# The head of a three-stage kernel: gate weights as 128x32 tiles, loads in another order, four banks, and the softmax split among other work

## The reference, cut to what matters

```python
# 1: pooled attention over q, k, v: (8, 8, 576, 64), k and v averaged over 8 neighbouring rows
scores = scale * q @ k_p.T;  attn = softmax(scores);  x = attn @ v_p      # x as (4608, 512)
# 2: gated product with w1, w2 (512 x 1024), w3 (1024 x 1024), w_out (1024 x 512)
a = x @ w1;  b = x @ w2
x = (a * b @ w3) @ w_out
# 3: routed experts: 8 experts, w1 (512 x 1024), w2 (1024 x 512) each
logits = x @ w_gate + modality_bias[modality_id]                          # w_gate (512 x 8)
e_idx = argmax(logits);  gate_w = the softmax's largest value
out[mask e] = gate_w * (relu(x[mask e] @ w1[e]) @ w2[e])
```

## Time and profile before

| | us |
|---|---|
| median of 3 runs | 1252.79 (1251.92 to 1253.19) |
| the profiled execution's own time | 1254.1 |
| its span, first to last instruction | 1252.3 |
| first matmul of the head | 7.24 |
| first product with w1, end of the head | 98.86 |
| PE busy | 1213.1 (97% of the span) |
| DVE, ACT, POOL busy | 549.8, 284.3, 207.5 |

### The profile page before, as it was taken

How to read it: one execution, slowest core, us unless ns; L and a number is a source line. 1 busy time by engine, 2 the same in 40 slices (tenths; PEclk the granted TensorE clock), 3 DMA queues, 4 the chain that set the end, 5 groups by cost and what they waited for, 6 DMA issues and landing times.

```text
span 1252.3 us, 26312 instructions
## 1 busy us (share of the span) xinstructions
PE 1213.1 (97%) x10372; PEld 1158.8 (93%) x10373; DVE 549.8 (44%) x1299; ACT 284.3 (23%) x647; POOL 207.5 (17%) x242
## 2 busy tenths in 40 slices
PE   7899999999999999999999999999999999999996
PEld 6789989999999999999999999989989989999995
DVE  2774655636546546557455143542222234222221
ACT  2432222312222312222222123311211122111110
POOL 1333012102210111121020000022112112112121
PEclk9989999999999999999999999999999999999998
DMA  5752103213223023022030004025111111111111
GB/s 206 267 174 83 71 36 92 81 44 82 85 67 119 27 83 108 19 86 95 27 100 1 36 1 168 27 68 185 51 42 52 40 34 52 34 42 59 34 51 34
DMA packets 41812, 92.75 MB, mean 74 GB/s; under 512 B 9587, under 2 KB 16755, under 8 KB 40692
## 3 DMA queue, kind: packets, MB, share of 16 engines
q1 hardware_dynamic: 32868, 66.68, 16.1%
q0 software_dynamic: 6400, 20.50, 5.1%
q10 hardware_dynamic: 2448, 4.21, 1.1%
HBM read 70.88 MB, written 21.01 MB: 73 GB/s over the span
## 4 chain that ended last, share of the span: by engine, by line
PE 93%; DVE 3%; DMA 2%; issue 1%; ACT 1%; POOL 0%; ACTq 0%; POOLq 0%; SPq 0%; DVEq 0%
PE ab L720 17%; PE ab L721 17%; PE ab L722 17%; PE x2p L720 6%; PE rt L720 6%; PE x2p L722 6%; PE x2p L721 6%; PE rt L722 6%; PE rt L721 6%; PE sct L774 3%; PE ab L796 2%; PE sct L855 1%; PE ab L737 1%; DMA qt<-in_q 1%; DMA w_raw<-in_moe_w 0%
## 5 line engine op out<-in xcount | busy, mean ns | idle before, releaser
L720 PE MATMUL ab<-xth,e1h 128*128 128x256 f32 x608 | 170.3, 280 | 2.1 <-DVE xtl L1406 2.1
L721 PE MATMUL ab<-xtl,e1h 128*128 128x256 f32 x608 | 171.3, 282 | 0.0
L722 PE MATMUL ab<-xth,e1l 128*128 128x256 f32 x608 | 170.1, 280 | 0.0
L720 PE MATMUL ab<-xh,w1h 128*128 128x288 f32 x512 | 154.0, 301 | 3.5 <-issue 2.0
L720 PE MATMUL ab<-xh,w2h 128*128 128x288 f32 x512 | 150.8, 294 | 0.0
L721 PE MATMUL ab<-xl,w2h 128*128 128x288 f32 x512 | 150.8, 294 | 0.0
L721 PE MATMUL ab<-xl,w1h 128*128 128x288 f32 x512 | 150.8, 294 | 0.0
L722 PE MATMUL ab<-xh,w1l 128*128 128x288 f32 x512 | 150.8, 294 | 0.0
L722 PE MATMUL ab<-xh,w2l 128*128 128x288 f32 x512 | 150.7, 294 | 0.0
L1246 DVE TENSOR_TENSOR ac<-ab,ac 128x288 f32<-128x288 f32 x128 | 58.2, 455 | 192.6 <-ACT ac L1039 191.1
L1039 ACT ACTIVATE ac<-ab 128x288 f32<-128x288 f32 x128 | 52.6, 411 | 338.4 <-PE ab L722 335.5
(11 more groups left out here) (202 smaller groups left out, 2711.5 us busy)
## 6 DMA issues: line engine op xcount, KB each, us to landing
kv<-in_v SPq DMA_DIRECT2D x24, 512.0 KB, 4.9
qt<-in_q SPq DMA_DIRECT2D x8, 1280.0 KB, 5.6
kv<-in_k SPq DMA_DIRECT2D x16, 576.0 KB, 7.2
x_rows<-xr SPq DMA_DIRECT2D x36, 256.0 KB, 3.2
stage<-in_moe_w SPq DMA_DIRECT2D x8, 1024.0 KB, 13.3
vp<-v_rows SPq DMA_DIRECT2D x32, 192.0 KB, 3.5
w_raw<-in_moe_w ACTq DMA_DIRECT2D x16, 256.0 KB, 4.6
wo_raw<-in_moe_w_out SPq DMA_DIRECT2D x8, 256.0 KB, 7.5
```

What stands on the lines that cost most here:

```text
L720: pe.matmul(outp, lh, rh, start=first, stop=False)
L721: pe.matmul(outp, lh, rl, start=False, stop=False)
L722: return pe.matmul(outp, ll, rh, start=False, stop=last)
```

## The change

Seven things change, all in the head.

1. w_out @ w_gate is turned round: w_gate, widened with zeros to 32 columns, becomes the stationary side (128x32, one such tile in each of the four column groups, `ab0[32n:32n+32]`), and the transposed w_out moves in 512 columns (`wog_turned`, 8 matmuls). The four partial sums of each half are copied to `wog_t` (one half by ACT, one by DVE), and 8 matmuls against a 0/1 matrix `fold` (made by POOL) add and transpose them (`wog`).
2. Chunk 0 is made without gate columns (260 and 252 columns); its 8 gate columns come later, by 24 matmuls of 128x8 (`lg0`), with a split of their own (`hi_lg0`, `lo_lg0`). For that chunk 0's w3 is kept in buffers of its own (`w3th0`, `w3tl0`). The first score round waits for `lo_lg0`, whose bank it uses.
3. The parts go through four banks instead of three: a part waits for the part four before it.
4. w_out is loaded whole, then its transpose in four transfers; q follows k without a wait; the pieces 0 to 3 of w1, w2 come behind the small tables. The two w3 loads of chunk 1 are issued behind the first splits on ACT's queue.
5. The score round of chunk `c` stands ahead of its first half, not between its halves.
6. DVE does `lo_w34` of the chunk before between `soft_max` and `soft_sum`, and `lo_w3t` between `soft_sum` and `soft_turn`.
7. `lo_w12` of pieces 0 and 1 stands ahead of the first round, of 2 and 3 in chunk 7; `hi_w12` goes along one a chunk.

```diff
-W12_WITH = [[], [0, 1], [2, 3], [4], [5], [6], [7], []]
...
-START_ROUND = {2: 0, 3: 1, 4: 2, 5: 3, 6: 4}
...
-        wo_t = at("wo_t", 48 * KB, [P, FC, KC, P], F32)
+        wo_t = at("wo_t", 48 * KB, [P, 2, KC, 512], F32)
+        w3th0 = at("w3th0", 64 * KB + 4 * XW * 4, [P, FC, P], F32R)
+        w3tl0 = at("w3tl0", 64 * KB + 4 * XW * (FC + 4), [P, FC, P], F32R)
+        wog_t = at("wog_t", 64 * KB + 4 * XW * 2, [P, 2, 512], F32)
...
-            engine.dma_start(wo_t[:, f, :, :], w_out_t[f]).then_inc(wot_in[f], 16)
+        def load_wo_t(engine, half):
+            for n in range(0, KC, 2):
+                engine.dma_start(wo_t[:, half, n:n + 2, :], w_out_t[:, half, n:n + 2, :]).then_inc(wot_in[half], 16)
...
-        def start_bank(n):
-            return (x2p[:, 0:XH], ab1[:, 1, 0:XH], rt[:, 0:XH])[n % 3]
+        def start_bank(c, part):
+            bank = (ab1[:, 0, :], ab1[:, 1, :], x2p, rt)[(2 * c + part) % 4]
+            return bank[:, 0:DM - XH] if c == 0 and part else bank[:, 0:XH]
+
+        def w34_cols(c, part):
+            return slice(XH * part, DM if c == 0 and part else XH * (part + 1))
+
+        def w3_parts(c):
+            return (w3th, w3tl) if c else (w3th0, w3tl0)
         def x2_bank(n):
             return (x2p, rt)[n % 2][:, 0:XH]
-        wps = ab0[:, 0, 0:FC * E]
+        wps = sct[:, 0, 0:FC * E]
+        lps = sct[:, 1, 0:E]
...
-                if f:
-                    load_wo_t(sp, f - 1)
-            load_wo_t(sp, FC - 1)
+            load_wo_t(sp, 0)
+            load_wo_t(sp, 1)
             load_k(0, 0)
             load_k(0, 1)
-            for n in range(2):
-                sp.wait_ge(w3t_ready, 3 + n)
-                for c in range(2 * n, 2 * n + 2):
-                    load_w12(sp, c)
             load_q(0)
...
+            for c in range(W12_DVE):
+                load_w12(sp, c)
...
-                cols = slice(XH * part, XH * (part + 1))
+                cols = w34_cols(c, part)
+                hi, lo = w3_parts(c)
                 for f in fs:
-                    if c == 0:
+                    if c == 0 and part == 0:
                         pe.wait_ge(w3tl_ready, f // 4 + 1)
                         pe.wait_ge(wo_lo_ready, f + 1)
-                    mm = split(start_bank(2 * c + part), w3th[:, f, :], w3tl[:, f, :], wo_hi[:, f, cols],
+                    mm = split(start_bank(c, part), hi[:, f, :], lo[:, f, :], wo_hi[:, f, cols],
                                wo_lo[:, f, cols], f == 0, f == FC - 1)
                 return mm
-            def wog(f):
-                pe.wait_ge(wot_in[f], 16)
-                for n in range(KC):
-                    mm = pe.matmul(wps[:, E * f:E * (f + 1)], wo_t[:, f, n, :], wg[:, n, :], start=(n == 0),
-                                   stop=(n == KC - 1))
-                return mm
+            def wog_turned():
+                pe.wait_ge(wg_in, 16)
+                for half in range(2):
+                    pe.wait_ge(wot_in[half], 32)
+                    for n in range(KC):
+                        mm = pe.matmul(ab0[Q * n:Q * (n + 1), half, :], wg[:, n, :], wo_t[:, half, n, :],
+                                       start=True, stop=True)
+                    mm.then_inc(wog_t_done, 1)
+
+            def wog():
+                pe.wait_ge(fold_made, 5)
+                for f in range(FC):
+                    if f % 4 == 0:
+                        pe.wait_ge(wog_t_taken[f // 4], 1)
+                    mm = pe.matmul(wps[:, E * f:E * (f + 1)], wog_t[:, f // 4, P * (f % 4):P * (f % 4 + 1)],
+                                   fold[:, :], start=True, stop=True)
+                mm.then_inc(wog_done, 1)
+
+            def lg0():
+                for f in range(FC):
+                    mm = split(lps, w3th0[:, f, :], w3tl0[:, f, :], wo_hi[:, f, DM:XW], wo_lo[:, f, DM:XW],
+                               f == 0, f == FC - 1)
+                mm.then_inc(lg0_done, 1)
             def first_w34():
-                pe.wait_ge(wg_in, 16)
-                for f in range(FC):
-                    mm = w34_part(0, 0, [f])
-                    if f:
-                        wog(f - 1)
-                mm.then_inc(w34_done, 1)
-                wog(FC - 1).then_inc(wog_done, 1)
+                w34_part(0, 0, range(FC)).then_inc(w34_done, 1)
+                w34_part(0, 1, range(FC)).then_inc(w34_done, 1)
+                wog_turned()
+                pe.wait_ge(w3tl_ready, 3)
+                w34_part(1, 0, range(0, 4))
+                wog()
+                pe.wait_ge(w3tl_ready, 4)
+                w34_part(1, 0, range(4, FC)).then_inc(w34_done, 1)
                 pe.wait_ge(wog_lo_ready, 1)
-                w34_part(0, 1, range(0, 4)).then_inc(w34_half, 1)
-                w34_part(0, 1, range(4, FC)).then_inc(w34_done, 1)
+                w34_part(1, 1, range(0, 4)).then_inc(w34_half, 1)
+                w34_part(1, 1, range(4, FC)).then_inc(w34_done, 1)
+                lg0()
             def mul_w34(c, half):
                 pe.wait_ge(w3tl_ready, 2 * c + half + 1)
                 for part in range(2):
-                    if half == 0 and 2 * c + part >= 3:
-                        pe.wait_ge(w34h_ready, 2 * c + part - 2)
-                        pe.wait_ge(w34l_ready, 2 * c + part - 2)
+                    if half == 0:
+                        pe.wait_ge(w34h_ready, 2 * c + part - 3)
+                        pe.wait_ge(w34l_ready, 2 * c + part - 3)
...
+                else:
+                    pe.wait_ge(lg0_lo_ready, 1)
...
-            for c in range(1, FC):
+            for c in range(2, FC):
+                if c < FC - 1:
+                    score(0, c - 2)
                 mul_w34(c, 0)
-                if c in START_ROUND:
-                    score(0, START_ROUND[c])
                 if c == FC - 1:
                     weigh_v(0, 0)
                 mul_w34(c, 1)
...
-            for half in range(2):
-                load_w3(act, 1, half)
...
             hi_wo(0)
+            load_w3(act, 1, 0)
             copy_w3t(0, 1)
+            load_w3(act, 1, 1)
             for f in range(1, FC):
                 hi_wo(f)
             hi_w34(0, 0)
+            copy_w3t(1, 0)
+            copy_w3t(1, 1)
+            hi_w34(0, 1)
+            act.wait_ge(wog_t_done, 1)
+            act.activation(wog_t[:, 0, :], ab0[:, 0, :], ACT.Copy).then_inc(wog_t_taken[0], 1)
             hi_wog()
-            for c in range(FC):
-                if c + 1 < FC:
+            hi_w34(1, 0)
+            copy_w3t(2, 0)
+            hi_w34(1, 1)
+            copy_w3t(2, 1)
+            hi_lg0()
+            hi_w12(0)
+            hi_w12(1)
+            for c in range(2, FC):
+                if c > 2:
+                    copy_w3t(c, 1)
+                    if c == FC - 1:
+                        hi_w12(c)
+                    hi_w34(c - 1, 0)
+                    hi_w34(c - 1, 1)
+                if c < FC - 1:
+                    exp_p(0, c - 2)
                     copy_w3t(c + 1, 0)
-                if c in START_ROUND:
-                    exp_p(0, START_ROUND[c])
-                if c == FC - 1:
+                    hi_w12(c)
+                else:
                     hi_x(0, 0)
-                for part in range(0 if c else 1, 2):
-                    hi_w34(c, part)
-                if c + 1 < FC:
-                    copy_w3t(c + 1, 1)
-                for n in W12_WITH[c]:
-                    hi_w12(n)
+            hi_w34(FC - 1, 0)
+            hi_w34(FC - 1, 1)
...
             lo_w34(0, 0)
+            lo_w3t(1, 0)
+            lo_w3t(1, 1)
+            lo_w34(0, 1)
+            dve.wait_ge(wog_t_done, 2)
+            dve.tensor_copy(wog_t[:, 1, :], ab0[:, 1, :]).then_inc(wog_t_taken[1], 1)
             lo_wog()
-            for c in range(FC):
-                s = START_ROUND.get(c)
-                if s == 0:
-                    dve.wait_ge(pad_stored, 32)
-                if s is not None:
-                    soft_max(0, s)
-                if c + 1 < FC:
+            lo_w34(1, 0)
+            lo_w3t(2, 0)
+            lo_w34(1, 1)
+            lo_w3t(2, 1)
+            lo_lg0()
+            lo_w12(0)
+            lo_w12(1)
+            dve.wait_ge(pad_stored, 32)
+            for c in range(2, FC):
+                if c > 2:
+                    lo_w3t(c, 1)
+                if c < FC - 1:
+                    soft_max(0, c - 2)
+                if c > 2:
+                    lo_w34(c - 1, 0)
+                    lo_w34(c - 1, 1)
+                if c < FC - 1:
+                    soft_sum(0, c - 2)
                     lo_w3t(c + 1, 0)
-                if s is not None:
-                    soft_sum(0, s)
-                    soft_turn(0, s)
-                if c == FC - 1:
+                    soft_turn(0, c - 2)
+                else:
+                    lo_w12(2)
+                    lo_w12(3)
                     lo_x(0, 0)
-                for part in range(0 if c else 1, 2):
```

(15 more changed lines are left out.)

42 lines of the change are left out of this document (30 added, 12 removed).

## The result

Five runs of the changed kernel gave a median of 1245.15 us (1244.67 to 1246.85), five of the kernel before 1252.79. The ratio is 0.9943, its 95% interval 0.9931 to 0.9955: faster by 7.6 us, a third of the 22.0 that were forecast, and outside the range. The profiled execution took 1246.85 us with a span of 1245.1.

What follows compares the result with a forecast made beforehand. Only the 98.86 us head, with PE's waits and slow clock, could give time. Prologue to 28.6, five rounds 34.0, DVE lateness 2, end 12.3 make 76.9: 22.0 us less, median 1230.8; forecast 1228.5 to 1235, range 1225 to 1240.

Steps and rivals of the forecast that it cites:

- One count in the working: Prologue loads: w_out's piece 7 at most the 12th transfer instead of the 19th, 6.7 fewer, reaching ACT at 12.1 us.
- The rival of a late prologue: Prologue: wog_turned's tiles run one behind another, or the clock stays 1.2 GHz, or both; 1233 to 1239 us, chance 0.14.
- so the whole gain stays: Behind the head: everything waits for things shifted alike, so all 22.0 us won in the head remain.
- costs PE 2: Softmax rounds: of DVE's 6.3 us of lateness, 0 to 3.8 reaches PE, taken as 2; chunk 7 starts at 64.6.
- the tail: End of the head, chunk 7's start to the first product with w1: 10.7 us plus 1.6 for DVE's lateness, 12.3.
- 2.3 for a late start: First round: DVE starts 2.3 us behind PE, because lo_w12 of two pieces stands ahead of it.
- the slack: Rounds: DVE's work of 6.4 us is 0.4 less than PE's 6.8, so five rounds regain 5 x 0.4 us.
- DVE becomes the bound: Rounds stay at 8.33 us, the head ends at 82.6, gain 16.3, 1236.5 us; chance 0.13.
- the low end of its bounds: Prologue, lg0's 24 matmuls of 8 columns: 1.4 to 2.9 us, taken as 1.9 because only the stationary load is left.

Runs made afterwards that it cites:

- w2l_moved: Changed kernel with POOL's four late w2 subtractions moved to other times, the whole computation kept: 1237.04 us, 0.9874 of the kernel before.
- v_held: Changed kernel with SP holding batch 3's loads of v until PE finished the first product behind its loop's entry: 1244.63 us, ratio 0.9935.
- late_part1: Changed kernel without a separate product for chunk 0's gate columns; its part 1 (260 columns) runs behind chunk 1's part 0: 1236.14 us, ratio 0.9888.

## Why the prediction was wrong

**Where it held.** Part 0 of chunk 0 ended at 14.4 us (forecast 14.0), the clock had risen by then, part 1 ended at 17.3 (16.8). One count in the working is off: by the order of SP's queue 6 pieces of the transpose, not 7, stand ahead of w_out's last piece, which makes the forecast 0.7 us too early. `wog_turned` took 2.02 us, as forecast. Its 16 records of 512 columns are 4060 record-columns a us, where a lone fp32r stream moves 260 columns in 0.12 us, 2170 a us, so column groups do run side by side. The Trainium skill (TensorE: Matmul & The Clock Gate, Part 3) gives 3.07 times for four packed row tiles, by which these column tiles would take an estimated 2.6 us. The measured 2.02 us stands against carrying that figure over. q and k came in time, and four banks took the waits of the chunk parts for a free bank away, as forecast. The rival of a late prologue is out, though the first scores came at 30.26, 1.7 us behind the forecast.

**First failed step: "so the whole gain stays".** It treated what lies behind the head as a chain that only shifts. Semaphores do shift alike; the arrival of PE's own code does not. The change leaves PE with 23 instructions fewer, which puts the loop's start 12 instructions ahead of the end of a fetched piece. Cost: 6.3 us at one place. No rival had this, although "issue" stood in the trace of before at this very jump (2.03 us), and the waits of the whole span would have shown it.

**Second failed step, a term mis-sized: DVE's lateness "costs PE 2" in the rounds and 1.6 in the tail.** The mechanism was named: POOL's exclusion of two-input DVE instructions. It was priced as 1.5 us in each of three rounds, 1.5 for the pooling of v and 2.3 for a late start, together 6.3 us of lateness once the slack is taken off, of which PE would feel 2 in the rounds and, with the 0.5 of an undisturbed tail, 1.6 behind them. Measured are 2.2 us in each of three rounds (2.94 less 0.75), 1.3 on a `lo_w3t` (2.03 less 0.69) and 1.2 on the two `lo_w12` (3.56 less 2.36), 9.1 us in all. Before that, beside the pooling of v, DVE's first two rounds took 7.99 and 7.73 us from `soft_max` to `soft_max`, 3.3 more than twice 6.19. The slack was there, and larger than the 0.4 us a round that were forecast: 0.8, DVE's 6.19 in PE's 7.00. It is far less than 2.2. PE stood 2.5 us for `lo_w3t` and 3.3 ahead of `weigh_v`, and the low clock behind the latter cost some 2.5 more, which had no term at all. Taking POOL's hold away gives 9.4 us back, of which 0.4 had been there since the first scores (29.81 in w2l_moved, 30.26 in after). So the rival "DVE becomes the bound" was the true case (it forecast a head end of 82.6; 86.84 came), with POOL's hold as the reason and not DVE's own work.

**Third, small and partly cancelling.** `lg0` took 2.6 us and not 1.9, near one matmul each 0.11 us: I had put it near the low end of its bounds, and it lay near the high one. Behind it came a round at a granted clock of 0.80, 1.5 us longer; the prediction had no term for a fall of the clock in the rounds. A round is 7.00 us and not 6.8. Against these, the tail is shorter: in w2l_moved chunk 7 starts at 66.34 (forecast 64.6) and the head ends 11.1 us later (forecast 12.3), at 77.43, 0.5 from the forecast's 76.9.

**The balance.** 22.0 forecast, less 9.4 (POOL's hold), less 0.5 (the rest of the head), less 6.3 (second stall), plus some 2 that came back behind it, is 7.8; the spans differ by 7.2 and the medians by 7.6.

**Not settled.** Whether traffic makes the second stall longer is not shown: v_held left the traffic at that place as it was, and no other run held it back. That the clock falls behind `lg0` because its matmuls are narrow is argued, not shown alone: in late_part1, which has none, the fall comes later, behind a wait for `lo_w3t`.

## What to carry to other kernels

Before a change that adds or removes instructions on the bound engine, look for "issue" waits where its code jumps back: count the instructions between such waits over two or three versions, and move the loop's start (a few cheap instructions ahead of it) if a piece ends right behind it. Set a hold by another engine against the slack of a round: here 2.2 us against 0.8, three times over, and the waits that came of it cost clock on top. Look at which instruction the hold will meet in the new order, not at its length in the old one. Check that an edit meant to hold a transfer back moves it at the place in question: v_held moved the same line of code 175 us too early. A stretch "that only shifts" should be checked by its length: here 1153.4 before, 1158.1 after, 1152.9 with both causes mended.

## What the runs showed of the hardware that was not expected

PE's instructions arrive in pieces of 256, each one packet of an instruction queue (71 packets, 1.16 MB in after's span). After the jump back PE stands 1.4 to 2.0 us, and a second time, 1.7 to 4.5 us, if the first piece ends within 12 matmuls; PE goes on 1.15 to 1.41 us behind the landing of the next piece. 22 instructions more ahead of the loop made the changed kernel some 7 us faster, 22 fewer made the one before 3.1 us slower although its head was 2.35 us shorter. Four fp32 column tiles of 128x32 take 2.02 us for 16 records of 512 columns. Matmuls of 8 columns follow at 0.11 us, hardly faster than those of 260 columns at 0.12.
